# The second layer's gate computed on VectorE from token rows instead of on TensorE, with the second routing over 24 tiles of tokens

## What is computed

```python
x = attention(q, k, v)                      # (3072, 512)
# first MoE: each token goes to its best expert, scaled by its gate
logits = x @ w_gate + modality_bias[modality_id]
e_idx = argmax(logits, axis=1)
out[mask] = gate_w[mask, None] * (relu(x[mask] @ w1[e]) @ w2[e])
# second MoE: x is the first one's output
logits = x @ w_gate2                        # (3072, 8)
order = argsort(-logits.flatten())
for idx in order:                           # greedy, 384 tokens per expert
    if assigned[tok] >= 0 or counts[e] >= cap: continue
    assigned[tok] = e; counts[e] += 1
out[mask] = relu(x[mask] @ w1b[e]) @ w2b[e]
```

## Time and profile before

| | us |
|---|---|
| median of 3 runs | 1154.97 |
| lowest and highest | 1146.36 and 1155.27 |
| the profiled execution | 1148.96 |
| its span, first to last instruction | 1146.9 |
| its mean granted TensorE clock | 0.937 of 2.4 GHz |

### The profile page before, as it was taken

One profiled execution on the slowest core, in us unless ns is written; L12 is line 12 of the kernel. 1 busy time (PEld: TensorE's weight loads), 2 busy tenths in 40 slices (PEclk: granted clock), 3 DMA queues, 4 the chain that ended last, 5 costly groups with the idle time before them and its releaser, 6 DMA issues.

```text
span 1146.9 us, 22896 instructions
## 1 busy us (share of the span) xinstructions
PE 1011.8 (88%) x7214; PEld 867.6 (76%) x7215; DVE 489.9 (43%) x1488; ACT 460.8 (40%) x1034; POOL 491.7 (43%) x462
## 2 busy tenths in 40 slices
PE   5999999997599999989999983369999999988796
PEld 4899888986488888878888863357878787787685
DVE  3766767676511122231122237854755546440000
ACT  4767676765322222242222230123434343343441
POOL 7454444441120000140000140437776687877882
PEclk9999999998599999999999995569999999998998
DMA  8556565651531111151111110423243332335300
GB/s 208 146 136 158 139 154 132 152 137 35 205 144 37 37 37 37 37 183 37 37 37 37 37 37 1 172 77 102 102 159 118 130 103 101 111 106 183 107 28 28
DMA packets 57403, 113.57 MB, mean 99 GB/s; under 512 B 6672, under 2 KB 23056, under 8 KB 57360
## 3 DMA queue, kind: packets, MB, share of 16 engines
q1 hardware_dynamic: 51280, 92.98, 26.6%
q0 software_dynamic: 6080, 19.98, 5.5%
HBM read 91.37 MB, written 21.57 MB: 98 GB/s over the span
## 4 chain that ended last, share of the span: by engine, by line
PE 49%; POOL 14%; issue 13%; DMA 8%; DVE 7%; ACT 4%; DVEq 4%; POOLq 1%; SPq 0%; ACTq 0%
DMA out<-sb_rows_out,sb_tokens_at 6%; PE ps_bank L855 5%; PE ps_bank L837 4%; PE ps_bank L839 4%; PE ps_bank L838 4%; PE ps_bank L856 4%; POOL sb_w2l L566 4%; PE ps_bank L857 4%; POOL sb_hl L634 4%; PE ps_bank L727 3%; PE ps_bank L716 3%; PE ps_bank L744 2%; PE ps_bank L746 2%; PE ps_bank L762 2%; DVEq L1241 2%
## 5 line engine op out<-in xcount | busy, mean ns | idle before, releaser
L1442 DVE TENSOR_TENSOR sb_hl<-ps_bank,sb_hh 128x512 fp32r<-128x512 f32 x52 | 35.7, 687 | 227.8 <-ACT sb_hh L1111 227.8
L555 POOL COPY sb_gather_at<-sb_slot_token_i 128x1 int32 (+1 forms) x27 | 4.9, 182 | 278.6 <-PE ps_bank L816 278.6
L1041 ACT ACTIVATE sb_probs<-sb_masked,sb_neg_max 128x260 f32<-128x260 f32 (+1 forms) x192 | 94.4, 492 | 67.0 <-DVE sb_neg_max L1228 63.9
L566 POOL TENSOR_TENSOR sb_w2l<-sb_w_raw,sb_w2h 128x1024 fp32r<-128x1024 f32 x44 | 107.5, 2453 | 16.3 <-ACT sb_w2h L1097 16.3
L518 POOL TENSOR_TENSOR sb_kl<-sb_k_raw,sb_kh 128x768 fp32r<-128x768 f32 x32 | 58.6, 1833 | 122.2 <-ACT sb_kh L1054 122.1
L984 PE MATMUL ps_bank<-sb_xh,sb_w1h 128*128 128x384 f32 x256 | 97.0, 379 | 9.9 <-ACT sb_h L1167 7.9
L623 POOL TENSOR_TENSOR sb_w1l<-sb_w_raw,sb_w1h 128x1024 fp32r<-128x1024 f32 x32 | 75.6, 2378 | 39.3 <-ACT sb_w1h L1092 39.2
L1228 DVE CUSTOM_DVE_ANT_0 sb_masked<-ps_bank,sb_mask 128x260 f32<-128x260 f32 (+1 forms) x192 | 75.8, 401 | 34.4 <-PE ps_bank L716 31.4
L837 PE MATMUL ps_bank<-sb_w1h,sb_xh 128*128 128x512 f32 x208 | 83.4, 401 | 7.9 <-DVE sb_w1l L1431 6.2
L855 PE MATMUL ps_bank<-sb_w2h,sb_hh 128*128 128x512 f32 x208 | 86.3, 415 | 3.7
L985 PE MATMUL ps_bank<-sb_xl,sb_w1h 128*128 128x384 f32 x256 | 89.0, 348 | 0.0
(11 more groups left out here) (298 smaller groups left out, 2706.6 us busy)
## 6 DMA issues: line engine op xcount, KB each, us to landing
sb_w_raw<-w1b SPq DMA_DIRECT2D x8, 2048.0 KB, 8.7
sb_w_raw<-w2b SPq DMA_DIRECT2D x8, 2048.0 KB
sb_q_raw<-qT SPq DMA_DIRECT2D x64, 192.0 KB, 3.6
sb_k_raw<-kT SPq DMA_DIRECT2D x64, 192.0 KB, 3.8
y_rows<-sb_y_out SPq DMA_DIRECT2D x34, 258.0 KB, 2.4
sb_v<-v_tiles SPq DMA_DIRECT2D x32, 192.0 KB
x_rows<-sb_x_pair SPq DMA_DIRECT2D x16, 384.0 KB, 3.7
sb_w_raw<-w1a SPq DMA_DIRECT2D x3, 2048.0 KB, 8.8
```

What stands on the lines that cost most here:

```text
L566: pool.tensor_tensor(w2_part(w2l, p), w2_part(raw2, p), w2_part(w2h, p).bitcast(F32), ALU.subtract).then_inc(w2_lo[m], 1)
L1041: act.activation(probs[g % 2][:, 0:width(g)], masked_scores[g % 2][:, 0:width(g)], ACT.Exp, bias=neg_max[g % 2][:], scale=-1.0, accum_out= ...
```

## The change

The gate of the second MoE is taken off PE. `gate_rows(t)` on DVE reads the y rows of tile t-1 (tokens on partitions, 512 values each) and multiplies them with each of the eight gate columns, which SP loads as rows copied to all partitions (`wg_rows`); each of the eight instructions writes its products to a PSUM bank and their sum to one column of `logits_row`. It stands ahead of `low_h1(t, 0)`. The transposes of y, `gate_y`, `copy_y_t` and `keep_logits` go.

POOL now scatters the y rows and the logits rows to DRAM in token order; the rows of empty slots go to spare places behind the 3072. SP reads the logits back as 24 tiles when all are stored. The second routing therefore runs over NT = 24 tiles, without a mark for empty slots, and its row numbers are token numbers, so that POOL uses them for the gather and for the output. `choice2` is laid out by tile. The stores that cleared rows 24 to 31 of `y_rows` at the start go.

In the second MoE `low_x` moves from POOL to DVE for all experts, reading PSUM, and ACT's unrounded copy of x goes. For the last two experts `low_h` moves to DVE too, with ACT's second copy. POOL issues the gather for expert k+1 before its last two `low_h`, no longer waits for landed outputs (ACT does, two outputs later), and its and ACT's loops are written out. `step_places` is changed (its first entry from 0 to 3), and the row transposes stand at places 8, 9 and 14 of the down product, at 5, 6 and 8 in expert 5, and at 3, 5 and 7 in expert 6.

The diff, cut to its core:

```diff
+            for e in range(E):
+                sp.dma_start(wg_rows[:, e], wg2[e:e + 1].to_broadcast([P, DM])).then_inc(wg_loaded, 16)
...
-                first, end = order_of(sp, e, FIRST, END)
-                with sp.Fori(first, end) as t:
-                    sp.wait_ge(y_copied, t + 2)
-                    sp.wait_ge(token_put, t + 2)
-                    sp.dma_start(y_dram[bass.ds(t * P, P)], y_rows[:]).then_inc(y_stored, 16)
+            tiles, = order_of(sp, E - 1, END)
+            sp.wait_ge(l_stored, tiles * 16 + 32)
+            settle(sp)
+            sp.dma_start(logits2[:], l_dram[0:N].rearrange("(p t) e -> p t e", t=NT)).then_inc(logits2_loaded, 16)
...
+            def put_rows(at):
+                pool.indirect_dma_start(out=y_dram, out_offset=bass.IndirectOffsetOnAxis(ap=at, axis=0), in_=y_rows[:],
+                                        in_offset=None).then_inc(y_stored, 16)
+            def put_logits(at):
+                pool.indirect_dma_start(out=l_dram, out_offset=bass.IndirectOffsetOnAxis(ap=at, axis=0),
+                                        in_=logits_row[:], in_offset=None).then_inc(l_stored, 16)
+            def note_places(t):
+                pool.wait_ge(y_stored, t * 16 + 16)
+                pool.wait_ge(l_stored, t * 16 + 16)
+                settle(pool)
+                pool.tensor_copy(put_at[:], out_i[:, bass.ds(t, 2)])
+                pool.tensor_copy(gather_at[:], slot_token_i[:, bass.ds(t + 2, 1)]).then_inc(at_copied, 1)
+                pool.wait_ge(at_copied, t + 2)
+            def fetch_x(t):
+                pool.wait_ge(xp_ready, t + 1)
+                settle(pool)
+                pool.indirect_dma_start(out=x_rows[:, 0:DM], out_offset=None, in_=x_dram,
+                                        in_offset=bass.IndirectOffsetOnAxis(ap=gather_at[:, 0:1], axis=0)
+                                        ).then_inc(gathered, 16)
+                pool.wait_ge(gathered, t * 16 + 16)
+            def scatter_logits(t):
+                pool.wait_ge(logits2_kept, t + 2)
+                settle(pool)
+                put_logits(put_at[:, 0:1])
+            def scatter_y(t):
+                pool.wait_ge(y_copied, t + 2)
+                settle(pool)
+                put_rows(put_at[:, 1:2])
...
+            put_rows(out_i[:, 0:1])
+            put_logits(out_i[:, 0:1])
...
-                    gather_x(t + 2)
+                    note_places(t)
+                    scatter_logits(t)
+                    fetch_x(t + 2)
+                    scatter_y(t)
...
-            def low_x(k, i):
-                pool.wait_ge(x2_hi, k * CT + i + 2)
-                cols = slice(i * P, (i + 1) * P)
-                pool.tensor_tensor(xl[:, :, cols], x32[:].rearrange("p (c n) -> p c n", c=DC),
-                                   xh[:, :, cols].bitcast(F32), ALU.subtract).then_inc(x2_lo, 1)
...
-            def landed(k, i):
-                pool.wait_ge(out_stored, (k * CT + i) * 16 + 16)
-                settle(pool)
-                pool.memset(spare_pool[:, i:i + 1], 0.0).then_inc(scattered, 1)
...
+            def expert(k, last):
                 for f in range(FC):
-                    low_h(k, f)
+                    if f == FC - 2 and not last:
+                        gather(k + 1)
+                    if k < FREE:
+                        low_h(k, f)
                     if f < WP:
                         low_w2(1, k, f)
                 if not last:
-                    gather(k + 1, 1 - a)
                     low_w1(k + 1, 0)
                     low_w1(k + 1, 1)
-                    keep_tokens(k + 1, 1 - a)
                     low_w1(k + 1, 2)
-                scatter(k, a, 0)
+                scatter(k, 0)
                 if not last:
-                    low_x(k + 1, 0)
                     low_w1(k + 1, 3)
-                    low_x(k + 1, 1)
-                landed(k, 0)
-                scatter(k, a, 1)
-                if not last:
-                    low_x(k + 1, 2)
-                landed(k, 1)
-                scatter(k, a, 2)
-                landed(k, 2)
-            with pool.Fori(0, E // 2 - 1) as kk:
-                for a in range(2):
-                    expert(kk * 2 + a, a, False)
-            expert(E - 2, 0, False)
-            expert(E - 1, 1, True)
+                scatter(k, 1)
+                scatter(k, 2)
...
-            def gate_y(t):
-                pe.wait_ge(y_t_ready, t + 1)
-                pe.wait_ge(logits2_kept, t + 1)
-                for c in range(DC):
-                    mm = pe.matmul(gate_ps[:, 0:E], y_t[:, c], wg2_sb[:, c], start=(c == 0), stop=(c == DC - 1))
-                mm.then_inc(logits2_ready, 1)
...
-                    pe.wait_ge(y_copied, t + 1)
-                    transpose_rows(yt_ps, y_rows, yp_ready)
                     pe.wait_ge(gathered, t * 16 + 32)
                     transpose_rows(x_ps, x_rows, xp_ready)
                     transpose_h(t, 1)
+                    pe.wait_ge(y_copied, t + 1)
                     down_product(t, e)
-            tiles, = order_of(pe, E - 1, END)
-            pe.wait_ge(y_copied, tiles + 1)
-            transpose_rows(yt_ps, y_rows, yp_ready)
-            gate_y(tiles)
...
-                for t in range(half * MT // 2, (half + 1) * MT // 2):
-                    mm = pe.matmul(r_ps[0:TRIES[s], 0:E], passed[:, t, 0:TRIES[s]], choice2[:, :, t],
-                                   start=(t == 0), stop=(t == MT - 1))
+                for t in range(half * NT // 2, (half + 1) * NT // 2):
+                    mm = pe.matmul(r_ps[0:TRIES[s], 0:E], passed[:, t, 0:TRIES[s]], choice2[:, t],
+                                   start=(t == 0), stop=(t == NT - 1))
...
-            step_places = [0, 1, 5, 8, 10, 14, 17, 19, 24, 25, 27, 29, 31, 33, 34, 36, 38, 39, 41, 46, 51]
+            step_places = [3, 4, 7, 9, 10, 14, 16, 17, 22, 23, 24, 25, 28, 30, 31, 33, 35, 36, 38, 43, 50]
...
-                if step == STEPS - 4:
+                if step == STEPS - 2:
                     transpose_in(0, 0)
-                if step >= STEPS - 2:
-                    transpose_in(0, step - (STEPS - 3))
+                    transpose_in(0, 1)
+                if step == STEPS - 1:
+                    transpose_in(0, 2)
                 route(1, step)
             with pe.Fori(0, E // 2 - 2) as kk:
                 for a in range(2):
-                    expert_products(kk * 2 + a, a, True, False)
-            expert_products(E - 4, 0, True, False)
-            expert_products(E - 3, 1, False, False)
-            expert_products(E - 2, 0, False, False)
-            expert_products(E - 1, 1, False, True)
+                    expert_products(kk * 2 + a, a, True, (8, 9, 14))
+            expert_products(E - 4, 0, True, (8, 9, 14))
+            expert_products(E - 3, 1, False, (5, 6, 8))
+            expert_products(E - 2, 0, False, (3, 5, 7))
+            expert_products(E - 1, 1, False, ())
...
-                act.wait_ge(yp_ready, t + 1)
+                act.wait_ge(logits2_kept, t + 2)
...
-                act.copy(xh[:, :, i * P:(i + 1) * P], h2_ps[i % 2][:].rearrange("p (c n) -> p c n", c=DC))
-                act.copy(x32[:], h2_ps[i % 2][:]).then_inc(x2_hi, 1)
+                act.copy(xh[:, :, i * P:(i + 1) * P], h2_ps[i % 2][:].rearrange("p (c n) -> p c n", c=DC)
+                         ).then_inc(x2_hi, 1)
             def high_h(k, f):
                 act.wait_ge(h2_ready, k * FC + f + 1)
-                act.wait_ge(h2_lo, k * FC + f + 1)
                 hp = h2_ps[f % 2][:, 0:NB]
-                act.activation(hh[:, f], hp, ACT.Relu)
-                act.activation(h32[f % 2][:], hp, ACT.Relu).then_inc(h2_hi, 1)
-            def copy_y(k, a, i):
+                if k < FREE:
+                    act.wait_ge(h2_lo, k * FC + f + 1)
+                    act.activation(hh[:, f], hp, ACT.Relu)
+                    act.activation(h32[f % 2][:], hp, ACT.Relu).then_inc(h2_hi, 1)
+                else:
+                    act.activation(hh[:, f], hp, ACT.Relu).then_inc(h2_hi, 1)
...
+            def gate_rows(t):
+                dve.wait_ge(y_copied, t + 1)
+                dve.wait_ge(l_stored, t * 16 + 16)
+                settle(dve)
+                for e in range(E):
+                    if e % 2 == 0:
+                        dve.drain()
+                    gated = dve.tensor_tensor_reduce((r_ps, s_ps)[e % 2][:], y_rows[:], wg_rows[:, e], 1.0, 0.0, ALU.mult,
+                                                     ALU.add, logits_row[:, e:e + 1])
+                gated.then_inc(logits2_kept, 1)
...
+                    gate_rows(t)
                     low_h1(t, 0)
-                    copy_y_t(t)
                     low_x1(t + 1)
                     low_h1(t, 1)
-                    dve.wait_ge(y_stored, t * 16 + 16)
-                    dve.tensor_copy(y_rows[:, DM:DM + 1].bitcast(I32), slot_token_i[:, bass.ds(t, 1)]
-                                    ).then_inc(token_put, 1)
```

(29 more changed lines are left out.)

297 lines of the change are left out of this document (151 added, 146 removed).

## The result

The changed kernel took **1121.62 us** (median of 4 runs, 1118.45 to 1123.61), the kernel before 1151.35 us (4 runs, the three from before the change and one more, 1146.36 to 1155.27): ratio 0.9741, 95% interval 0.9688 to 0.9795. Faster, as forecast, and at almost the forecast time (1119). But the sum is right because its terms erred in both directions. The span fell from 1146.9 to 1119.5 us, by 27.4 us.

| stretch | before, us | after, us | difference | forecast |
|---|---|---|---|---|
| first product of the first layer to the start of the last write of y | 375.5 | 388.7 | +13.2 | +5.6 |
| end of that write to the first operation on the logits | 3.4 | 11.6 | +8.1 | +9.0 |
| the two lone routings | 67.2 | 57.6 | -9.6 | -10.8 |
| experts 0 to 4 | 250.9 | 227.0 | -23.9 | -16.1 |
| experts 5, 6, 7 | 48.5, 45.2, 35.3 | 43.7, 40.9, 33.2 | -11.2 | -17.5 |

A forecast was written before the change was run, and what follows sets the result against it. PE was taken to bound the kernel. From 1148.96 us, terms of -21.1, +26.7, +9.0, -14.3, -12.6 and -17.5 sum to -29.8, giving 1119 us; range 1092 to 1146.

The forecast's parts named there:

- First layer, what goes: First-layer tiles: gate products leave PE, 0.81 us in each of 26 tiles; removed y transposes worth nothing; 21.1 us gained.
- First layer, what comes: First-layer tiles: eight DVE gate passes, 5.5 us, fit into 5.63 us; 0 lost (0 to 0.5 us a tile).
- rival B: First-layer tiles: gate passes hold up PE in every tile, and half the last experts' gain is missing; 1140 us, chance 0.16.
- First layer, where an expert begins: Three expert starts: passes alternate with POOL's low_w2, PE idles and its clock falls; 26.7 us lost (bounds 0 and 30).
- Rival A: First-layer expert starts: DVE keeps the port through all passes, costing 9 us rather than 26.7; 1101 us, chance 0.15.
- Between the layers: Last y written to first routing operation: passes, scatter and load take 12.2 us, not 2.9; 9 us lost (7 to 13).
- The two lone routings: Routings outside the experts, plus expert 0's first wait: shorter operations over fewer tiles; 14.3 us gained (10 to 18).
- Routed experts: Experts with routing beside them: shorter counts give 9 us, vanished compare waits 3.6; 12.6 us gained (8 to 18).
- The last three: Experts 5, 6, 7: fewer PE waits, at 42.6, 35.2 and 33.8 us; 17.5 us gained (10 to 22).
- The end: Last product to the end of the span: forecast counted no change, 0 us.
- C: Gate passes: two SBUF inputs and an accumulator run at half rate, 1.15 us a pass; 1235 us, chance 0.10.
- D: Routing and expert stage: no speed-up, as other steps replace those shortened; 1150 us, no change, chance 0.07.

The follow-up runs named there:

- thin_low_w2: Changed kernel with POOL computing only 32 of 1024 elements of each low part of w2 in the first layer, from the second expert on: 1103.83 us.
- gather_early: Changed kernel with POOL issuing the gathers for experts 6 and 7 earlier: 1112.41 us, ratio 0.9685 to the kernel before.
- late_gates: Changed kernel with the gate passes behind both low halves of h and low x, and POOL's gather ahead of the logits scatter: 1093.63 us.
- ten_passes: Changed kernel with the gate passes for experts 0 and 1 done twice in each tile, ten in place of eight: 1190.36 us.

## Why the prediction was right or wrong

**First layer, what goes.** Right. The doubled products cost 0.89 us a tile (0.81 forecast), the doubled transposes 0.05 (0 forecast), and without passes the tile is 13.10 us (13.15 forecast).

**First layer, what comes.** This step failed, and with it more than half of the gain of the step before. The window was right (5.61 measured, 5.63 worked out). What went into it was not: the sum gave 5.5 us where it is 5.83, since it took 0.61 for every pass, where the second of a pair has 0.65, and 0.16 for a drain, which no row showed, where 0.25 stands between two pairs. Nothing was put down for DVE to start after ACT, 0.31 us. The rate was sound: the row named for it gives 1.19 ns an element by plain division (1.22 us for 1024), not 1.04, but the first pass of a pair does take 0.62 us. Still, a sum by 1.19 would have given 5.8 us and no fit, and the text gave no such upper bound. So the passes are 0.53 us late where the text had 0.1 us to spare. Its bound (0 to 0.5 a tile) and rival B's premise named this; 23 intervals gained 0.34 us each, 7.9 in place of 18.6. By the text's own test (a tile not under 13.6 us) the forecast was wrong here, if by a hair: most tiles take 13.60 to 13.64. A fit with 2% to spare should have been read as no fit.

**First layer, where an expert begins.** The mechanism was right: one pass for each operation of POOL, passes up to 2.9 us, PE idle up to 9.4, and its clock at the 1.2 GHz level behind that (a granted clock of 0.50 from 514 to 520 us). Rival A is out, by the trace and by `thin_low_w2`. The three starts lost 10.6 + 6.1 + 4.4 = 21.1 us against the kernel before, in spite of the 0.81 gained in each: 23.6, against 26.7 forecast. The distribution was off. The first start cost 11.4 in place of 7.5, since no pass was done before POOL began: the first started at 313.46, 1.17 us behind POOL's first. At the other two the text forgot that the 3.40 us row would go, as POOL comes to `low_w2` only behind its new scatter: DVE's four low parts of w1 take 4.63 us, not 6.80.

The Trainium skill (SBUF — State Buffer, "Who interferes with whom") has it that a DVE instruction with two SBUF inputs contends with a GpSimd instruction that reads SBUF, and calls the shared ports an exclusive lock. The traces agree (2.6 to 2.9 us for a pass of 0.7 beside POOL's operation of some 2.4), and add that with both queues full they take turns.

**Between the layers.** Right: 8.1 us against 9. The sizes of the parts were off in both directions: the load took 1.9 us, not 3.4, and the passes were done 6.3 us after y was written, not 5.5.

**The two lone routings.** Right: 9.6 against 10.8. (The terms of the second routing, 4.6 + 1.1 + 2.5 - 1.8, give 6.4, not 6.2.)

**Routed experts.** Mis-sized: with expert 0, 23.9 us in place of 16.1. For experts 1 to 4, 197.01 us with PE busy for 191.56 became 179.60 with PE busy for all of it. The waits gave 5.4 and the busy time 12.0, where 7.2 was forecast for shorter counts. Part of that rest is the clock: two of these experts had a granted clock of 0.97 before, with PE busy for 48.6 to 48.7 us, the other two 1.00 and 47.1 to 47.2; all have 1.00 and 44.9 now. So the counts gave 2.2 to 2.3 an expert, and the clock some 3 us in all. I counted the waits that go, and left out what they had cost behind them.

**The last three.** This step failed by 6.3 us: expert 6 took 40.9 us, not 35.2 (expert 5: 43.7 for 42.6, expert 7: 33.2 for 33.8). What failed is "the gather issued during the up product" as a reason for no wait: in expert 6 it is issued there, but behind four `low_w2`. PE starts the transposes at 1062.20, 7.4 us after the last issue at 1054.77, and they stand only three places into the down product:

```profile
1054.77 0.95 POOL L647 DMA_INDIRECT sb_rows_in<-y_rows,sb_slots_i  x1 [0.30 <-issue]
...
1062.20 1.12 PE L824 MATMUL ps_bank<-sb_ident,sb_rows_in 128*128 128x128 f32 x4 [3.96 <-DMA sb_rows_in<-y_rows,sb_slots_i]
```

`gather_early` takes the wait away and gives 34.45 us. By the text's own test (expert 6 over 40) the forecast was wrong on this point too.

**The end.** Left out: 4.1 us, half of them from POOL's wait for the last landing.

**Rivals.** C is out: a pass with both inputs in SBUF has a pitch of 0.62 to 0.65 us for 512 elements, no slower for an element than the custom pass out of PSUM. The Trainium skill (Vector Engine (DVE) Microarchitecture Reference, "Points that are easy to get wrong") states half throughput for one instruction form with two SBUF sources other than bf16. The trace doesn't name the form of this pass; the pass itself shows no halving, and for it the measurement decides. D is out: the routings and the experts did speed up, by 9.6 and 23.9 us. B was half true: the passes gate PE in every tile, and a part of the last experts' gain is missing. Without the 12 us that the routed experts and the end gave beyond the forecast, the time would have been 1133, between the forecast and B. The time fell close to the forecast by that compensation, which is luck: +7.6, -0.9, +1.2, -7.8, +6.3 and -4.1 against the terms, in the order of the table.

## What to carry to other kernels

When work moves to an idle engine, ask what stands behind it in that engine's queue: here the eight passes cost a steady tile nothing when they stood behind the one small operation that PE waits for. Their place ahead of it cost 28 us, which a change of order on DVE and POOL gave back. Work that nobody needs for a whole period belongs behind work that is needed at once. Count a start-up gap and the drains into a fit, and treat a fit with a few per cent to spare as none. Before a wait can go, follow the request in its own queue to the landing, not only the place in the code from which it is issued.

## What the runs showed of the hardware that was not expected

- Beside a long GpSimd operation DVE passes with two SBUF inputs went one for one: 2.6 to 2.9 us a pass in place of 0.7. Small operations of POOL pay the same way: its copy of one column beside a pass took 0.70 us (in the changed kernel, at 408.99), and 0.18 when DVE's passes stood elsewhere (`late_gates`, at 398.23).
- The price of PE's wait isn't its length alone. 1.1 us in every tile left the clock at full speed; 2.6 us in a tile (`ten_passes`) was followed in 19 of 23 tiles by some eight matmuls 0.43 us apart (granted clock 0.50, the 1.2 GHz level), 1.6 us more.
- A gather of three times 128 rows that was issued 2.0 us earlier landed only 0.8 us earlier (`gather_early`, expert 5).
